# Row maxima of an attention head turned on VectorE and moved by a DMA, in place of five TensorE transposes; chunks of the maxima and one emptying moved

## What is computed

```python
q_pool = q.reshape(B, H, S // 2, 2, D).mean(axis=3)
scores = scale * np.matmul(q_pool, k.transpose(0, 1, 3, 2))
scores = scores - np.max(scores, axis=-1, keepdims=True)
attn = np.exp(scores)
attn = attn / (np.sum(attn, axis=-1, keepdims=True) + 1e-09)
x = np.matmul(attn, v)                # then heads side by side: 1152 x 512
h = x @ w_in                          # 512 -> 2048
g = h * np.tanh(softplus(h))
x = g @ w_out                         # 2048 -> 512
h = x @ w2_in
g = np.where(h > 0, h, np.exp(np.minimum(h, 0)) - 1)
out = g @ w2_out
```

## Time and profile before

| | |
|---|---|
| median of 3 runs | 716.6 us (716.28 to 717.03) |
| profiled execution, its own time | 715.77 us |
| its span, first to last instruction | 714.0 us |
| attention (until about) | 303 us |
| PE busy / weight loads | 671.0 us (94%) / 648.5 us (91%) |
| DVE, ACT, POOL busy | 440.8 us (62%), 400.4 us (56%), 424.8 us (60%) |
| mean granted TensorE clock | 0.988 of 2.4 GHz |

### The profile page before, as it was taken

How to read it: one execution, slowest core, us unless ns; L and a number is a source line. 1 busy time by engine, 2 the same in 40 slices (tenths; PEclk the granted TensorE clock), 3 DMA queues, 4 the chain that set the end, 5 groups by cost and what they waited for, 6 DMA issues and landing times.

```text
span 714.0 us, 12393 instructions
## 1 busy us (share of the span) xinstructions
PE 671.0 (94%) x4064; PEld 648.5 (91%) x4064; DVE 440.8 (62%) x695; ACT 400.4 (56%) x743; POOL 424.8 (60%) x390
## 2 busy tenths in 40 slices
PE   3799999999999999999997999999999999999998
PEld 2788888888888888999997999999999999999998
DVE  7777878787878787477777556777543332223222
ACT  1587888788888787765555545655543322222221
POOL 3576777787878785568786666788644422222221
PEclk9799999999999999999998999999999999999999
DMA  7455555555555552011220000212222110001001
GB/s 200 129 143 139 139 154 140 140 140 140 143 136 156 128 149 60 16 45 59 60 63 12 0 0 15 60 60 60 61 69 74 50 45 0 0 0 45 0 1 45
DMA packets 30383, 54.86 MB, mean 77 GB/s; under 512 B 4480, under 2 KB 11904, under 8 KB 30336
## 3 DMA queue, kind: packets, MB, share of 16 engines
q1 hardware_dynamic: 30336, 54.25, 28.3%
HBM read 40.37 MB, written 2.36 MB: 60 GB/s over the span
## 4 chain that ended last, share of the span: by engine, by line
PE 78%; DVE 15%; issue 3%; POOL 1%; ACT 1%; DMA 1%; SPq 0%; POOLq 0%; ACTq 0%
PE py L488 10%; PE py L489 9%; PE py L490 9%; PE pH L473 9%; PE pH L474 9%; PE pH L475 9%; DVE part_max L712 8%; PE ps L388 5%; DVE pl L721 5%; PE ps L389 4%; PE pm L363 4%; PE po L404 3%; PE po L405 3%; PE po L406 3%; PE ps L371 2%
## 5 line engine op out<-in xcount | busy, mean ns | idle before, releaser
L1002 POOL TENSOR_TENSOR gl<-fg,gh 128x384 fp32r<-128x384 f32 x96 | 97.6, 1016 | 138.8 <-ACT gh L649 137.7
L712 DVE TENSOR_REDUCE part_max<-pm 128x1 f32<-128x384 f32 x231 | 125.5, 555 | 27.2 <-PE pm L363 20.1
L942 POOL TENSOR_TENSOR pl<-p,ph 128x576 fp32r<-128x576 f32 x72 | 106.3, 1481 | 59.2 <-ACT p L566 59.2
L488 PE MATMUL py<-gh,wout_h 128*128 128x384 f32 x384 | 129.8, 338 | 5.7 <-DVE xl L855 4.6
L489 PE MATMUL py<-gl,wout_h 128*128 128x384 f32 x384 | 129.1, 336 | 0.0
L490 PE MATMUL py<-gh,wout_l 128*128 128x384 f32 x384 | 129.1, 336 | 0.0
L473 PE MATMUL pH<-xh,win_h 128*128 (+1 forms) x384 | 128.7, 335 | 0.0
L474 PE MATMUL pH<-xl,win_h 128*128 (+1 forms) x384 | 128.5, 335 | 0.0
L475 PE MATMUL pH<-xh,win_l 128*128 (+1 forms) x384 | 128.5, 335 | 0.0
L560 ACT ACTIVATE ph<-ps 128x576 fp32r<-128x576 f32 x144 | 93.7, 651 | 46.6 <-PE ps L389 42.7
L834 DVE RECIPROCAL fi<-fp 128x192 f32<-128x192 f32 x48 | 64.9, 1353 | 52.6 <-POOL fp L1010 52.6
(11 more groups left out here) (71 smaller groups left out, 1398.0 us busy)
## 6 DMA issues: line engine op xcount, KB each, us to landing
k_raw<-kT SPq DMA_DIRECT2D x32, 288.0 KB, 4.3
w_raw<-w_in SPq DMA_DIRECT2D x32, 256.0 KB, 2.7
w_raw<-w_out SPq DMA_DIRECT2D x32, 256.0 KB, 2.6
q_raw<-qT SPq DMA_DIRECT2D x16, 288.0 KB, 3.2
k_pack<-kP SPq DMA_DIRECT2D x16, 288.0 KB, 2.7
v_raw<-v SPq DMA_DIRECT2D x16, 288.0 KB, 2.8
kl<-k_pack SPq DMA_DIRECT2D x32, 144.0 KB, 3.6
q<-q_hi SPq DMA_DIRECT2D x62, 72.0 KB, 2.3
```

The costliest lines, as they stand in the source:

```text
L488: pe.matmul(out, hi, gh[:, f % 4, :], start=(f == 0), stop=False)
L712: dve.tensor_reduce(part_max[:, par, t, c:c + 1], chunk_bank(j, par, first), AX.X, ALU.max).then_inc(m_read, 1)
```

## The change

1. `maxima_row` is gone on PE and ACT, and the identity matrix with it. `row_max` is 32 columns wide; after the last reduction DVE turns it with four transposes of 32 x 32 into `row_turned` (five rows of 128), and SyncE moves those into row 64 of `q2` with one DMA (`spread_row`). `kl` now holds minus ones in that row. `row_max` is written as fp32r. PE waits for this DMA (`row_spread`) before the first scores of a head. The score tiles of all heads alternate over the two tiles of `ps` without the extra turn.
2. The 15 chunks of a head are spread anew: four of them stand in steps 7 and 8 of the head before the previous one, eleven in steps 0 to 3 (3, 3, 3, 2). In head 0 there are 15 in steps 0 to 4, and 4 in steps 7 and 8.
3. `split_q` stands in step 2 on GpSimd in both kinds of head (before 3 and 2) and in step 1 on ACT (before 4 and 2), `copy_kh` in step 6 (before 7 and 6), `round_k` in step 5 (before behind `maxima_row`, at the same step).
4. In layer 0 `evacuate` and `low_y` stand in unit 2.

```diff
-MAX_STEPS = 5
+FIRST_CHUNKS = (3, 3, 3, 3, 3, 0, 0, 2, 2)
+CHUNKS = (3, 3, 3, 2, 0, 0, 0, 2, 2)
-GPSIMD_AT = {"sum_q": (0, 0), "split_q": (3, 2), "split_k": (6, 6), "split_v": (1, 1), "split_w": (4, 4),
+GPSIMD_AT = {"sum_q": (0, 0), "split_q": (2, 2), "split_k": (6, 6), "split_v": (1, 1), "split_w": (4, 4),
-SCALAR_AT = {"split_q": (4, 2), "split_v": (0, 1), "split_w": (3, 3)}
-VECTOR_AT = {"copy_kh": (7, 6), "invert": (4, None), "finalize": (6, None)}
+SCALAR_AT = {"round_k": (5, 5), "split_q": (1, 1), "split_v": (0, 1), "split_w": (3, 3)}
+VECTOR_AT = {"copy_kh": (6, 6), "invert": (4, None), "finalize": (6, None)}
...
+        def chunks_at(n, kt):
+            counts = FIRST_CHUNKS if n == 0 else CHUNKS
+            before = (0 if n == 0 else sum(CHUNKS[7:])) + sum(counts[:kt])
+            for j in range(before, before + counts[kt]):
+                head = n + 1 + j // NCH
+                if head < HEADS:
+                    yield head, j % NCH
...
+            def spread_row(m):
+                par = m % 2
+                sp.wait_ge(preset, par + 1)
+                sp.wait_ge(max_ready, m + 1)
+                sp.dma_start(q2[par][D:D + 1, :].bitcast(F32).rearrange("o (t c) -> o t c", c=P),
+                             row_turned[0:QT, par, :]).then_inc(row_spread, 16)
...
                 if not (isinstance(m, int) and m == 0):
                     for part, cols in ((top, slice(0, HQ)), (low, slice(HQ, SQ))):
                         move(q1[low, slot, cols], q_hi[part, :]).then_inc(q1_spread, 16)
                         move(q1[top, slot, cols], q_sum[part, :]).then_inc(q1_spread, 16)
+                if m > 0:
+                    spread_row(m - 1)
                 wait(sp, s_filled, slot_count(m - 2, KT - 1))
...
             for m in range(HEADS):
                 spread_head(m, m % 4, last=(m == HEADS - 1))
+            spread_row(HEADS - 1)
...
             def scores(n, kt, par, slot):
                 if kt == 0:
-                    wait_scored(pe, n, -2)
-                    wait(pe, s_read, slot_count(n, -1))
+                    wait(pe, row_spread, 16 * (n + 1))
                     wait(pe, kl_spread, 32 * (n + 1))
                     wait(pe, q2_spread, 32 * (n + 1))
-                else:
-                    wait_scored(pe, n, kt - 2)
+                wait_scored(pe, n, kt - 2)
...
-                        elif kt == KT - 1 - AHEAD:
-                            scores(*nxt, slot + par)
-                            pv(n, kt, par, slot + par, None if last else lambda: maxima_row(n + 1, 1 - par))
                         else:
-                            pv(n, kt, par, slot + par)
+                            pv(n, kt, par, slot + par, next_chunk)
                             if nxt is not None:
                                 scores(*nxt, slot + par + 1)
+                        next_chunk()
...
-                    late = f == (2 if layer else 3) and 0 <= tile < NT
+                    late = f == 2 and 0 <= tile < NT
...
                 if j == NCH - 1:
                     dve.wait_ge(m_read, NCH * (n + 1))
-                    dve.tensor_reduce(row_max[:, par, :], part_max[:, par, :, :], AX.X, ALU.max).then_inc(max_ready, 1)
+                    dve.tensor_reduce(row_max[:, par, 0:QT], part_max[:, par, :, :], AX.X, ALU.max).then_inc(row_reduced, 1)
+                    dve.wait_ge(row_reduced, n + 1)
+                    wait(dve, row_spread, 16 * (n - 1))
+                    for b in range(0, P, SQUARE):
+                        turn = dve.transpose(row_turned[:, par, b:b + SQUARE],
+                                             row_max[b:b + SQUARE, par, :].bitcast(F32))
+                    turn.then_inc(max_ready, 1)
```

More of the change, by code:

```diff
@@ L89, in build @@
             q1 = sa("q1", [P, 4, QP], F32R)
-            q2 = [sa(f"q2_{i}", [P, SQ], F32R) for i in range(2)]
+            q2 = [sa(f"q2_{i}", [P, QP], F32R) for i in range(2)]
             o_pair = sa("o_pair", [P, SQ])
@@ L364, in max_chunk @@
                           kh[par][:, c * MC:c * MC + MC], start=True, stop=True).then_inc(m_filled, 1)
[L366 to L373, removed]
             def scores(n, kt, par, slot):
                 if kt == 0:
-                    wait_scored(pe, n, -2)
-                    wait(pe, s_read, slot_count(n, -1))
+                    wait(pe, row_spread, 16 * (n + 1))
                     wait(pe, kl_spread, 32 * (n + 1))
                     wait(pe, q2_spread, 32 * (n + 1))
-                else:
-                    wait_scored(pe, n, kt - 2)
+                wait_scored(pe, n, kt - 2)
                 for half in range(2):
-                    out = ps[:, (1 + kt) % 2, half, 0:HQ]
+                    out = score_bank(n, kt)[:, half, 0:HQ]
                     q = slice(half * HQ, half * HQ + HQ)
@@ L426, in pair_step @@
                     n, last = 2 * p + par, is_last(p, par)
-                    chunks = iter(range(NCH))
-                    def next_chunk():
-                        max_chunk(n + 1, next(chunks), 1 - par, slot + par + 1)
                     for kt in range(KT):
@@ L437, in pair_step, with next_chunk @@
                         nxt = ahead(n, kt, par, last)
[L438 removed]
+                        chunks = chunks_at(n, kt)
+                        def next_chunk(chunks=chunks):
+                            for head, j in chunks:
+                                max_chunk(head, j, head % 2, head)
+                                break
+                        if kt + AHEAD < KT:
                             scores(*nxt, slot + par)
[L441 removed]
+                            next_chunk()
+                            if kt == 0:
                                 next_chunk()
[L443 to L455 removed]
+                            pv(n, kt, par, slot + par, next_chunk)
                         else:
[L457 removed]
+                            pv(n, kt, par, slot + par, next_chunk)
                             if nxt is not None:
                                 scores(*nxt, slot + par + 1)
+                        next_chunk()
             all_pairs(pair_step)
@@ L601, in pair_step @@
                             exp_tile(*nxt, slot + par + (kt + AHEAD >= KT))
-                        if kt + AHEAD == KT - 1 and not last:
-                            if is_first(p) and par == 0:
-                                act.wait_ge(preset, 2)
-                            maxima_row(n + 1, 1 - par)
-                            if not in_last_pair(p):
-                                round_k(n + 2)
                         at = lambda task: SCALAR_AT[task][par] == kt
@@ L610, in pair_step @@
                             split_v(n + 1, 1 - par)
+                        if at("round_k") and not in_last_pair(p):
+                            round_k(n + 2)
                         if at("split_w"):
@@ L787, in pair_step @@
                 for par in range(2):
-                    n, last, j = 2 * p + par, is_last(p, par), 0
+                    n, last = 2 * p + par, is_last(p, par)
                     for kt in range(KT):
-                        if not last:
-                            for c in range(3 if kt < MAX_STEPS else 0):
-                                if kt == 0 and c == 2:
-                                    late_split(p, n, par, slot)
-                                max_chunk(n + 1, j, 1 - par)
-                                j += 1
-                        elif kt == 0:
+                        for c, (head, j) in enumerate(chunks_at(n, kt)):
+                            if kt == 0 and c == 2:
+                                late_split(p, n, par, slot)
+                            max_chunk(head, j, head % 2)
+                        if last and kt == 0:
                             late_split(p, n, par, slot)
@@ L898, in _ @@
                     for f in range(4):
-                        late = f == (2 if layer else 3) and tile >= 0
+                        late = f == 2 and tile >= 0
                         unit_step(layer, t, f, base + f, 0, prior=tile if late else None)
```

61 lines of the change are left out of this document (21 added, 40 removed).

## The result

The changed kernel takes **752.96 us** (median of 4 runs, 752.17 to 754.89), the kernel before 716.44 (4 runs, 715.53 to 717.03). The ratio is 1.0515, with a 95% interval from 1.0492 to 1.0538: **36.5 us slower**. Forecast were 745.6 us, with a range from 722 to 771. The profiled execution's own time is 754.89 us.

What follows compares the result with a forecast made beforehand. PE was taken to bound the kernel, with the loop through GpSimd and SyncE's queue taking over; +30.0 + 1.6 - 0.9 - 5.7 + 4 = +29.0 us on 715.8 gave 744.8, 745.6 on the median, range 722 to 771.

Steps and rivals of the forecast that it cites:

- heads 1 to 14, without falls of the clock: Attention: periods of 20.3 us (six even heads) and 19.4 (seven odd), 257.6 against 227.6, +30.0 us.
- falls of the clock there: Attention, PE idle before first scores: the clock falls at two heads, +4 us; ends 0 and 31.
- head 0 to 1: Start of the attention: head 1's first scores at 42.6 us against 41.02, +1.6 us.
- head 14 to 15: Last attention heads: the row stands behind no queries, DVE's end counts, 16.5 us in place of 17.44, -0.9.
- from the first scores of head 15 on: Layer 0's emptying in unit 2: PE's first `xl` wait becomes 1.2 us without a clock fall, -5.7 us.
- The row is in time: Attention: `split_q` ends 12.3 us behind the first scores, so periods stay at 17.5; 690 us, chance 0.10.
- Dips all through the attention: Sign in the profile's clock row that would show the forecast to be wrong; no size given.
- the loop: Attention: first scores, exponentials, GpSimd's work, `split_q`, SyncE, DMA, first scores; periods of 20.3 and 19.4 us.
- my quick end: Low bound for the landing of the row's DMA, 2.0 us, where 2.3 was taken.
- the third rival: Attention: the clock falls at nearly every head, 2.2 us each, 31 us in place of 4; 772 us, chance 0.20.

Runs made afterwards that it cites:

- the matmuls ahead of the wait: The changed kernel with ten matmuls of 384 columns put before PE's wait for the row, heads 1 to 14: 746.76 us, ratio 1.0426.
- the row alone: The changed kernel without early chunks (15 in steps 0 to 4) and with the row's DMA ahead of the wait for `ql_done`: 730.77 us, ratio 1.0207.
- the spread division: The changed kernel with GpSimd's `split_q` in step 1 and DVE's division of a pair spread over both heads: 716.42 us, ratio 0.9998 against the kernel before.
- the early queries: The changed kernel with GpSimd's `split_q` in step 1, `split_v` and `multiply_sums` in step 2, `split_x` in step 3: 735.96 us, ratio 1.0272.

## Why the prediction was right

The sum, term by term, in the profiled execution (its time was 754.9 us, forecast 744.8):

| term | forecast | measured |
|---|---|---|
| heads 1 to 14, without falls of the clock | +30.0 | +29.5 (257.1 with the matmuls ahead of the wait) |
| falls of the clock there | +4 | +9.8 (266.9 less 257.1) |
| head 0 to 1 | +1.6 | +2.2 (43.20 against 41.02) |
| head 14 to 15 | -0.9 | +1.4 (18.81 against 17.44) |
| from the first scores of head 15 on | -5.7 | -3.7 (424.2 against 427.9) |
| span | +29.0 | +39.1 |

**The mechanism held.** The row stood behind `split_q`, one load and four moves; PE waited for it 14 times; the maxima were old by then, and so the transposes covered. "The row is in time", the faster rival, failed on GpSimd's end at 14.4 us (odd) and 15.9 (even, both at the full clock), where 12.3 were needed; moving `split_q` sooner did remove the wait. (To keep all of the gain it would have had to end by 17.5 - 1.34 - 5.2 = 11.0 us, not by 10.8.)

Two of the announced signs came out otherwise. "Dips all through the attention" was named as a sign of being wrong, and by the windows they are there: the clock falls in 9 of the 13 heads, though the page's row shows no more of them than a single 8 behind the start. And GpSimd does pause between its first low part and `split_q`, 1.67 and 0.70 us in head 6 and 0.67 and 0.27 in head 5, each time for ACT's exponentials. So the loop does not run through GpSimd's work alone: what comes late on PE and ACT makes `split_q` late as well.

**The loop's parts** were each a little off, and cancelled: that 30.0 came so close to 29.5 is luck. Behind `split_q` I had 5.2 us; it is 4.7 (159.24 to 163.95), since issue to scores took 1.81 where I put 2.4, below my quick end of 2.0 from the moves. No row had shown the 0.1 us for PE's wake-up by itself; it is within the 1.81. The Trainium skill ("DMA: Bandwidth & Descriptors", Anatomy of one DMA) has about 2.0 us, in a section on DMAs that GpSimd issues, while these are SyncE's; by it the 14 heads would have come out 4 us sooner, and the measurement went further in the same direction. The size of the DMA mattered little: 2.5 KB took 1.81 us to the start of the scores, 72 KB a median of 2.1 to 2.3 to landing.

Ahead of the queue, `split_q` ends in even heads at the full clock 15.9 us behind the first scores, not 15.1, in odd ones 14.4, not 14.2. For even heads I had offset the later block 4 by 0.4 us of slack; GpSimd begins its low part 10.15 us behind the first scores (62.48 to 72.63), against 8.46 before (128.59 to 137.05), so it came 1.7 later where I had 0.8. The four reductions ahead of `copy_sum` cost PE a visible wait, 8.8 us in 15 heads, 0.6 each.

**The clock term was mis-sized.** I took two falls; 9 of 13 heads show a lower mean clock. PE's waits were 1.3 to 2.8 us, 10 of the 14 between 2.2 and 2.4, not the 3 to 4 that I announced, and I had no row between 1.03 us (no fall) and 4.56 (a fall). What a fall costs on the path differs: an even head goes from 20.6 to 21.4 (once to 22.5), an odd one from 19.1 to between 20.2 and 21.0, and the first one shows no loss (19.20 us at 0.91). So the third rival's 2.2 us per head was too high, its frequency nearly right. The Trainium skill ("TensorE: Matmul & The Clock Gate", HAM oscillation) says of a kernel with longer waits than these that it drops at each of them; the traces agree in most heads, not in all. The 9.8 us are the difference of two profiled executions. Their medians differ by 6.2.

**Head 14 to 15.** I let DVE's end count. The row's DMA was issued at 325.96, so with 1.81 us it was there at 327.8, and PE came to the first scores at 328.95 without a wait for it. PE's own order behind a fall at 310.14 (mean clock 0.91) set the time. The fall is 0.8 of the 2.3 us that I was off: with the matmuls ahead of the wait, at the full clock, the same head took 18.0.

**Emptying.** The wait for the first `xl` fell from 4.56 us to 0.93 without a fall (forecast 1.2), as costed. But a wait that was not there before came at the first tile of layer 1:

```profile
424.77 0.34 PE L477 MATMUL pH<-xh,win_l 128*128 x1
426.04 0.44 PE L490 MATMUL py<-gh,wout_h 128*128 128x384 f32 x1 [0.93 <-DVE xl L851]
...
560.54 0.44 PE L490 MATMUL py<-gh,wout_h 128*128 128x384 f32 x1 [1.08 <-DVE xl L851]
```

ACT stands ahead of it for 1.77 us, until 558.09, waiting for a weight chunk from memory; its evacuation comes behind that. The emptying itself did not move there, it is in unit 2 of that tile in both kernels, and ACT waited for the same chunk before as well (1.51 us, until 516.52) without PE being held. What changed is the distance: from the first matmul behind the first `xl` to the one that needs the emptied bank PE would take 133.4 us now (426.04 to 560.54 less the wait of 1.08), where it took 135.7 (385.78 to 521.50), part of it at the low clock. ACT's chunk came after 132.1 us, against 130.7 before; why it came later stays open. By itself the emptying gives 4.9 us. I had looked at the tile whose wait went, not at what PE would be too early for further on.

## What to carry to other kernels

When a result changes from an engine's own work to a DMA, look at what stands ahead of that DMA in its queue and for whom the neighbours are needed: with two urgent users in one in-order queue, changing their order moved the wait and gained 7 us at best of the 36.5 lost; the gain had to come from making both inputs ready sooner. A new order on one engine also changes what it runs beside: look at the mean time of each instruction in every run, not at the waits alone. Shrinking work on the bounding engine pays only after the path beside it is shorter than the new period; here that took three steps on other engines, and only with the third was it faster than the kernel before (queries sooner, division away from GpSimd's work, sums ahead of a reduction). Where a short wait on PE recurs, count the clock as a cost of its own and read it head by head.

## What the hardware showed that I had not expected

**DVE against GpSimd.** A product on DVE with both inputs in SBUF took 0.78 us alone and 1.97 beside a GpSimd product. The instruction of DVE started at 156.75; GpSimd's, started at 156.68, ended at 158.11, and 0.76 us more give 158.87, near the measured end of 158.72. In turn GpSimd's next one, started at 158.07, took 1.91 in place of 1.43. The 2.05 in place of 1.43 in the earlier trace rows, which stood beside DVE's `copy_kh`, a copy with one input, is of the same size. The Trainium skill ("SBUF — State Buffer", Who interferes with whom) has this as a rule: a DVE instruction with two SBUF inputs and a GpSimd one that reads SBUF exclude each other for a whole instruction. The trace agrees with it for the products. The products were slow in other runs above as well: 1742 and 1648 ns on average with the row ahead of the queries, 822 and 1311 with the row before the moves, 822 and 1691 with the row alone, against 785 and 758 in the spread division. With the early queries alone the two products took 1739 and 1646 ns on average; the spread division sheds 8 x (0.95 + 0.89) = 14.7 us of DVE's time by that, and gained 19.5. Four heads of the kernel with the early queries also have a fall (mean clock 0.92), and none with the spread division. How much of the 19.5 came from that, and how much from the other places in the order, was not separated.

**The clock isn't set by the last wait alone.** Two waits of the same size, one ahead of a head at the full clock and one ahead of a head with a fall:

```profile
123.50 0.40 PE L400 MATMUL ps<-q,kh 128*128 128x288 f32 x1 [2.39 <-DMA q<-row_turned]
...
228.07 0.40 PE L400 MATMUL ps<-q,kh 128*128 128x288 f32 x1 [2.22 <-DMA q<-row_turned]
```

```profile
123.40:142.50 19.10, 15.76 (x105) 14.62 (x105) 14.54 (x28) 13.57 (x24) 15.84 (x12) 1.00 0.51 131
...
228.00:249.30 21.30, 17.31 (x105) 16.16 (x105) 16.21 (x30) 13.27 (x23) 10.59 (x9) 0.92 0.46 117
```

Behind 2.39 us of idling the engine stayed at 2.4 GHz, and behind 2.22 it fell to 1.2 for a while (granted clock 0.50 from 229 to 231 us). In the run with the row alone, the head behind a wait of 2.03 us kept the full clock (1.00), and one with waits of 1.48 and 1.45 us did not (0.92). Why the one and not the other stays open. Waits of 0.47 and 0.63 us at the same places, with matmuls ahead of them, left it at the full clock.

**A small transpose is a fifth of a microsecond.** 32 x 32 on DVE took 0.20 us each, 64 times within 4 ns, where I had estimated 0.17 from the small reduction.
